# Windowed attention and two feed-forward layers: which operand of the values product stands still, and a new order at both ends

## The chip, the cores and the metric

One core of a Trainium2 chip runs the whole program. The metric is the device time of one execution in microseconds (us). The engines are PE (products; PEld is its weight load), DVE, ACT and POOL (elementwise work) and SP, which issues the DMAs.

## The reference, cut to what matters

Inputs: q, k, v of 4 batches x 8 heads x 768 positions x 64; 8 memory keys and values; two feed-forward layers, 512 to 2048 to 512. All is float32.

```
for each chunk c of 32 queries:
    keys = 8 memory + 16 left + 32 own + 8 right   # 64; outside the sequence: absent
    a = exp(scale * q_c @ keys.T - rowmax);  a = a / (rowsum(a) + 1e-9)
    heads[:, :, c] = a @ values                    # 32x64 times 64x64
x = heads as 3072 x 512
h = x @ w_in;  y = max(0.01 h, h) @ w_out
h = y @ w_in2;  g = (a0 + a1 h + a2 h^2 + a3 h^3) / (1 + |b0||h| + |b1| h^2 + 1e-6)
out = g @ w_out2
```

## The kernel before

The 3072 rows are 8 tiles of 384 (TILE), each of three groups of 128 (GPT = 3), 24 groups in all. A group holds 4 chunks (cc) of 8 heads, as 2 sets (st) of 4 slots (j).

**Phase A** (`tile_a`, 8 tiles) is the first feed-forward layer with the attention of coming tiles woven in. Its step f makes one 128-row slice of the hidden layer: `gemm1` (12 products of 384 columns, L580 to L582: each operand is split in a high and a low part, three products make one), ACT scales (L778), DVE takes the maximum (L1013), ACT rounds to g_hi (L784), DVE subtracts for g_lo (L1016), and three steps later (LAG) `gemm2_a` takes it (L597 to L599). **Phase B** (`tile_b`) does the second layer likewise (`gemm2_b`, L615 to L617, 512 columns); its activation takes seven DVE operations a step (`step_b`; L1042, L1052 and L1063 end it), ACT rounds (L790), DVE makes g_lo (L1022), and `save_out` (L826) copies a tile's three outputs, which SP stores.

**Attention of one group** takes 32 score products (L503, L514), the softmax, 32 values products (L539, L552), and the heads' split into x_hi (ACT) and x_lo (DVE), the operands of `gemm1`. A float32 product of this form is two records of PE. In `values` (groups 6 to 23) the normalised probabilities, turned by DVE (L939), stand still, 64 keys x 32 queries, and the values move, 64 columns; the output has queries on partitions, so DVE turns it (`turn_values`, L963) before ACT (L767) and DVE (L968) split it:

```
nc.tensor.matmul(at.loop_values_at[CHUNK * j:CHUNK * (j + 1), st, :, cc, :],   # stays 64x32,
                 at.probs_t[DH * st:DH * (st + 1), q0:q0 + CHUNK],             # 8 places of the
                 v_of(ring(c), st, j, cc), start=True, stop=True)              # array in use
```

In groups 0 to 5 PE turns the probabilities (`transpose_probs`, L522), ACT copies them (L761), and the heads are normalised (L994) and turned (L1001) afterwards. Groups 3 to 5 (the early ones) go through the first tile's steps: scores at step f = 3, 7, 11, turned at f+1, values at f+2, saved at f+3. For later groups scores are at f = 15, 5, 10, values at 4, 9, 14, and the split at 5, 10, 14. The next group's scores wait for the last one's turned heads (`wait_scores`).

x_hi and x_lo have two halves. Tile t's result y is written into half t % 2 and stored to HBM from there (`store_y`, L351); `save_heads` waits for y_stored before the first group of a tile overwrites that half. POOL splits the weights that SP loads (L463, L466), two operations a half slice; `gemm1` and `gemm2_a` wait for them (`wait_weights`). ACT does the rounding of the first two slices (L877).

**The first tile** has an order of its own, written out at the end of each engine's block: three groups in three places of PSUM, with `keep_warm` products between them.

## Time and profile before

| | us |
|---|---|
| median of three runs (lowest, highest) | 1141.11 (1140.07, 1141.95) |
| the profiled execution | 1140.21 |
| its span | 1138.4 |
| the first layer's products, first to last start | 19.1 to 603 |
| `gemm2_b`, first to last start | 605.5 to 1134.9 |

Rows give start and length in us from the span's start. In rows of groups the numbers behind the bar are the busy time in us and the mean length of one instruction in ns. A product's record holds its passage through the array, so records overlap: what counts is the distance from start to start. `<-` names what ended an engine's idle time.

### The profile page before, as it was taken

To read this page: it belongs to the slowest core of one execution; us is meant where nothing else is said; L and a number is where in the kernel's file an instruction comes from. 1 tells how busy PE (TensorE), PEld (TensorE's weight loads), DVE (VectorE), ACT (ScalarE), POOL (GpSimd) and SP (SyncE) were. 2 spreads that over 40 slices of the span, in tenths; PEclk is the share of its full clock that TensorE was granted. 3 is DMA by queue.
4 is the path that set the end of the run, shared out by engine and by line. 5 is a ranking of instruction groups with operands and counts; after the bars stand their busy time and mean duration, and the time that the engine had idled before them with its cause. 6 is when DMAs were issued, how large, how long until landed. Compare 5 with 4: busy or idle time off the path is not lost.

```text
span 1138.4 us, 23079 instructions
## 1 busy us (share of the span) xinstructions
PE 1127.2 (99%) x8881; PEld 1057.2 (93%) x8881; DVE 784.2 (69%) x1512; ACT 587.8 (52%) x1423; POOL 129.4 (11%) x130
## 2 busy tenths in 40 slices
PE   7999999999999999999999999999999999999998
PEld 6999999999999999999999999999999999999996
DVE  6655555555556555554228888888888888888886
ACT  4323333333333334333237776767767677676765
POOL 3991211111211112000000000000000000000000
PEclk9999999999999999999999999999999999999999
DMA  7663525335352354300975020020202002020000
GB/s 263 206 198 116 195 76 185 104 129 197 112 186 102 109 181 149 139 1 14 356 251 194 1 84 1 2 82 1 84 1 84 1 1 84 1 84 1 29 1 28
DMA packets 43018, 114.78 MB, mean 101 GB/s; under 512 B 4897, under 2 KB 5025, under 8 KB 42913
## 3 DMA queue, kind: packets, MB, share of 16 engines
q1 hardware_dynamic: 42912, 113.33, 28.4%
q8 instruction: 71, 1.16, 0.4%
q14 instruction: 35, 0.28, 0.1%
HBM read 77.66 MB, written 35.65 MB: 100 GB/s over the span
## 4 chain that ended last, share of the span: by engine, by line
PE 96%; DVE 1%; DMA 1%; ACT 1%; issue 0%; SPq 0%; DVEq 0%
PE psum L582 15%; PE psum L580 15%; PE psum L581 15%; PE psum L597 8%; PE psum L616 8%; PE psum L617 8%; PE psum L598 8%; PE psum L599 8%; PE psum L615 8%; PE psum L539 1%; PE psum L503 1%; DMA spare<-groups_in 1%; DVE g_lo L1016 0%; PE psum L552 0%; PE psum L680 0%
## 5 line engine op out<-in xcount | busy, mean ns | idle before, releaser
L582 PE MATMUL psum<-x_hi,w_lo 128*128 128x384 f32 x1016 | 341.2, 336 | 0.0
L580 PE MATMUL psum<-x_hi,w_hi 128*128 128x384 f32 x1016 | 340.8, 335 | 0.3 <-DVE scratch L1013 0.3
L581 PE MATMUL psum<-x_lo,w_hi 128*128 128x384 f32 x1016 | 340.3, 335 | 0.0
L580 PEld LDWEIGHTS psum<-x_hi,w_hi 128*128 128x128 f32 x1016 | 190.8, 188 | 6.2 <-issue 0.6
L581 PEld LDWEIGHTS psum<-x_lo,w_hi 128*128 128x128 f32 x1016 | 190.7, 188 | 5.4
L1013 DVE TENSOR_TENSOR scratch<-psum,scratch 128x384 f32<-128x384 f32 x128 | 71.3, 557 | 178.9 <-ACT scratch L778 177.1
L582 PEld LDWEIGHTS psum<-x_hi,w_lo 128*128 128x128 f32 x1016 | 190.6, 188 | 0.0
L597 PE MATMUL psum<-g_hi,w_hi 128*128 128x384 f32 x512 | 176.1, 344 | 0.0
L598 PE MATMUL psum<-g_lo,w_hi 128*128 128x384 f32 x512 | 171.2, 334 | 0.0
L599 PE MATMUL psum<-g_hi,w_lo 128*128 128x384 f32 x512 | 171.1, 334 | 0.0
L778 ACT ACTIVATE scratch<-psum 128x384 f32<-128x384 f32 x128 | 63.5, 496 | 187.9 <-PE psum L582 182.3
L798 ACT ACTIVATE scratch<-psum,cf 128x384 f32<-128x384 f32 x128 | 74.6, 583 | 151.4 <-PE psum L582 151.4
L617 PE MATMUL psum<-w_hi,g_lo 128*128 128x512 f32 x384 | 152.0, 396 | 0.0
L616 PE MATMUL psum<-w_lo,g_hi 128*128 128x512 f32 x384 | 151.6, 395 | 0.0
L615 PE MATMUL psum<-w_hi,g_hi 128*128 128x512 f32 x384 | 149.5, 389 | 1.5 <-DVE g_lo L1022 1.5
L784 ACT CAST g_hi<-scratch 128x384 fp32r<-128x384 f32 x128 | 65.7, 513 | 137.0 <-DVE scratch L1013 135.5
L1036 DVE SCALAR_TENSOR_TENSOR scratch<-scratch,cf 128x384 f32<-128x384 f32 x128 | 79.2, 618 | 77.6 <-ACT scratch L799 77.6
L1016 DVE TENSOR_TENSOR g_lo<-scratch,g_hi 128x384 fp32r<-128x384 f32 x128 | 78.9, 617 | 74.2 <-ACT g_hi L784 74.2
L597 PEld LDWEIGHTS psum<-g_hi,w_hi 128*128 128x128 f32 x512 | 96.0, 188 | 4.2
L598 PEld LDWEIGHTS psum<-g_lo,w_hi 128*128 128x128 f32 x512 | 96.2, 188 | 0.0
L599 PEld LDWEIGHTS psum<-g_hi,w_lo 128*128 128x128 f32 x512 | 96.1, 188 | 0.0
L617 PEld LDWEIGHTS psum<-w_hi,g_lo 128*128 128x128 f32 x384 | 72.0, 187 | 15.4
(93 smaller groups left out, 1486.2 us busy)
## 6 DMA issues: line engine op xcount, KB each, us to landing
scratch<-groups_in SPq DMA_DIRECT2D x23, 768.0 KB, 6.7
raw<-weights_in SPq DMA_DIRECT2D x64, 256.0 KB, 4.3
scratch<-groups_in SPq DMA_DIRECT2D x23, 512.0 KB, 5.3
...
x_hi_scratch<-x_hi SPq DMA_DIRECT2D x8, 768.0 KB, 3.3
```

What stands on the lines that cost most here:

```text
L580: nc.tensor.matmul(bank, hi, x_hi[:, b, k, :], start=(k == 0), stop=False)
L581: nc.tensor.matmul(bank, hi, x_lo[:, b, k, :], start=False, stop=False)
L582: last = nc.tensor.matmul(bank, lo, x_hi[:, b, k, :], start=False, stop=(k == KT - 1))
L597: nc.tensor.matmul(bank, hi, g_hi[:, f % G_RING, :], start=(f == 0), stop=False)
L598: nc.tensor.matmul(bank, hi, g_lo[:, f % G_RING, :], start=False, stop=False)
L599: last = nc.tensor.matmul(bank, lo, g_hi[:, f % G_RING, :], start=False, stop=(f == NF - 1))
L615: nc.tensor.matmul(bank, hi, w_hi[:, f, 1, :], start=(f == 0), stop=False)
L616: nc.tensor.matmul(bank, hi, w_lo[:, f, 1, :], start=False, stop=False)
L617: last = nc.tensor.matmul(bank, lo, w_hi[:, f, 1, :], start=False, stop=(f == NF - 1))
L798: nc.scalar.activation(absb, h, ACT.Abs, scale=cf[:, 4:5])
L1016: nc.vector.tensor_tensor(g_lo[:, f % G_RING, :], leaky[f % 2], g_hi[:, f % G_RING, :].bitcast(F32), ALU.subtract).then_inc(g_lo_ready, 1)
L1036: nc.vector.scalar_tensor_tensor(quad[c], h2, cf[:, 6:7], absb, ALU.mult, ALU.add).then_inc(quad_ready, 1)
```

## The change

- **The values products** swap operands: the values stand still (64 keys x 64 columns) and the probabilities move (32 columns). The output has the model's dimension on partitions, as `gemm1` wants it, in 64-row halves, so four places of the array are in use where there were eight. `turn_values` and `turn_heads` are gone; ACT and DVE split straight from PSUM, in the step of the values product (f = 4, 9, 14). `wait_scores` now waits for x_ready. The host no longer permutes w_in's rows.
- **Softmax of groups 0 to 5**: probabilities, not heads, are normalised, before PE turns them; POOL does it for groups 0 and 1 ahead of its weight splits. ACT makes group 1's sums with its exponentials in place of group 2's. The early groups gain a step: scores f, normalise f+1, turn f+2, values and split f+3.
- **The start**: SP asks for the third group's values after three scores, and for weights after two exponentials; PE's order changes, nine warming products become three, and `first_gemm1` needs the low weight parts last. ACT rounds a weight slice on each side of the third group's cast.
- **The end**: the last slice's correction, activation, rounding and low part are done in two parts (256 and 128 columns), steps 14 and 15 are interleaved anew, `last_gemm2` starts on each part as it comes, and DVE copies the middle output.

The diff, cut:

```diff
-EARLY_TRANSPOSE = {f + 1: g for f, g in EARLY_SCORES.items()}
-EARLY_VALUES = {f + 2: g for f, g in EARLY_SCORES.items()}
-EARLY_SAVE = {f + 3: g for f, g in EARLY_SCORES.items()}
+EARLY_NORMALISE = {f + 1: g for f, g in EARLY_SCORES.items()}
+EARLY_TRANSPOSE = {f + 2: g for f, g in EARLY_SCORES.items()}
+EARLY_VALUES = {f + 3: g for f, g in EARLY_SCORES.items()}
 EARLY = 2 * GPT
...
     sp.wait_ge(qk_loaded[1], 16)
     load_v(0, 0)
     load_v(1, 1)
-    sp.wait_ge(probs_t_ready, 2)
+    sp.wait_ge(scores_ready, GPT)
     load_v(2, 2)
+    sp.wait_ge(exp_ready, 2)
     for j in range(RAW):
         load_raw(j, j, first=True)
...
-            sp.wait_ge(o_saved, GPT * t + j + 1)
+            if isinstance(t, int) and t == TILES - 1 and j == 1:
+                sp.wait_ge(o_saved_dve, 1)
+            else:
+                sp.wait_ge(o_saved, GPT * t + min(j + 1, saved_by_act(t)))
...
+    def normalise_first(g, at):
+        pool.wait_ge(sums_ready, 3 * g + 3)
+        nc.gpsimd.tensor_tensor(at.loop_probs, at.loop_probs,
+                                at.loop_inv.unsqueeze(2).broadcast_to([P, SETS * CPG, KEYS]),
+                                ALU.mult).then_inc(first_normalised, 1)
+    for g in range(BY_POOL):
+        normalise_first(g, first_att[g])
...
     def scores(c, at):
...
     def transpose_probs(g, at):
-        pe.wait_ge(exp_ready, g + 1)
+        if g < BY_POOL:
+            pe.wait_ge(first_normalised, g + 1)
+        else:
+            pe.wait_ge(normalised, g - BY_POOL + 1)
         for a in range(2 * SETS):
...
+                    r0 = DH * (j % 2)
                     last = nc.tensor.matmul(
-                        at.loop_values_at[CHUNK * j:CHUNK * (j + 1), st, :, cc, :],
-                        at.probs_t[DH * st:DH * (st + 1), q0:q0 + CHUNK],
-                        v_of(ring(c), st, j, cc), start=True, stop=True)
+                        at.loop_x[r0:r0 + DH, st, j // 2, CHUNK * cc:CHUNK * (cc + 1)],
+                        v_of(ring(c), st, j, cc),
+                        at.probs_t[DH * st:DH * (st + 1), q0:q0 + CHUNK], start=True, stop=True)
         last.then_inc(heads_ready, 1)
     def values_first(c, at):
         for st in range(SETS):
             for cp in range(2):
-                for c2 in range(2):
-                    for j in range(SLOTS):
+                for j in range(SLOTS):
+                    for c2 in range(2):
                         q0 = (st * 2 + cp) * P + j * CHUNK
+                        r0 = DH * (j % 2)
                         last = nc.tensor.matmul(
-                            at.values_at[CHUNK * j:CHUNK * (j + 1), c2, st, :, cp, :],
-                            at.probs_t[DH * c2:DH * (c2 + 1), q0:q0 + CHUNK],
-                            first_v_of(ring(c), st, j, cp, c2), start=True, stop=True)
+                            at.first_x[r0:r0 + DH, c2, 2 * st + j // 2, CHUNK * cp:CHUNK * (cp + 1)],
+                            first_v_of(ring(c), st, j, cp, c2),
+                            at.probs_t[DH * c2:DH * (c2 + 1), q0:q0 + CHUNK], start=True, stop=True)
         last.then_inc(heads_ready, 1)
...
             gemm2_a(n0 + f - LAG, f - LAG, t)
+    def last_gemm2():
+        f, r = NF - 1, (NF - 1) % G_RING
+        all_steps = STEPS_A + TILES * NF
...
+                                    start=False, stop=stop)
+        wait_weights(f, 1, True)
+        pe.wait_ge(g_hi_ready, all_steps)
+        product(0, g_hi, w_hi)
+        product(0, g_hi, w_lo)
+        pe.wait_ge(g_lo_ready, all_steps)
+        product(0, g_lo, w_hi, stop=True).then_inc(o_ready, 1)
+        product(1, g_hi, w_hi)
+        product(1, g_hi, w_lo)
+        product(1, g_lo, w_hi, stop=True).then_inc(o_ready, 1)
+        pe.wait_ge(g_hi_ready, all_steps + 1)
+        product(2, g_hi, w_hi)
+        product(2, g_hi, w_lo)
+        pe.wait_ge(g_lo_ready, all_steps + 1)
+        product(2, g_lo, w_hi, stop=True).then_inc(g_used, 1)
...
             for k in range(KT):
-                for w in (w_hi, w_lo):
-                    nc.tensor.matmul(psum[:, H_BANKS[f], 0:TILE], w[:, f, 0, P * k:P * (k + 1)], x_hi[:, 0, k, :],
-                                     start=(k == 0 and w is w_hi), stop=False)
+                nc.tensor.matmul(psum[:, H_BANKS[f], 0:TILE], w_hi[:, f, 0, P * k:P * (k + 1)], x_hi[:, 0, k, :],
+                                 start=(k == 0), stop=False)
         pe.wait_ge(x_ready, GPT)
         for f in (0, 1):
             for k in range(KT):
-                last = nc.tensor.matmul(psum[:, H_BANKS[f], 0:TILE], w_hi[:, f, 0, P * k:P * (k + 1)],
-                                        x_lo[:, 0, k, :], start=False, stop=(k == KT - 1))
+                nc.tensor.matmul(psum[:, H_BANKS[f], 0:TILE], w_hi[:, f, 0, P * k:P * (k + 1)], x_lo[:, 0, k, :],
+                                 start=False, stop=False)
+            wait_weights(f, 0, False)
+            for k in range(KT):
+                last = nc.tensor.matmul(psum[:, H_BANKS[f], 0:TILE], w_lo[:, f, 0, P * k:P * (k + 1)],
+                                        x_hi[:, 0, k, :], start=False, stop=(k == KT - 1))
             last.then_inc(h_ready, 1)
...
     pe.wait_ge(ident_loaded, 16)
     transpose_probs(0, first_att[0])
+    first_values(0)
     transpose_probs(1, first_att[1])
-    first_values(0)
+    transpose_probs(2, first_att[2])
     first_values(1)
-    transpose_probs(2, first_att[2])
     first_values(2)
-    keep_warm(9)
+    keep_warm(3)
     first_gemm1()
     for f in range(2, LAG):
...
     def save_heads(g, gi, b, at, t):
-        act.wait_ge(turned, g + 1)
+        act.wait_ge(heads_ready, g + 1)
         if gi == 0:
             act.wait_ge(y_stored, 32 * t + 1)
-        nc.scalar.copy(x_hi[:, b, :, P * gi:P * (gi + 1)], at.loop_heads).then_inc(xh_ready, 1)
+        to = x_hi[:, b, :, P * gi:P * (gi + 1)].rearrange("p (s u) n -> p s u n", s=SETS)
+        nc.scalar.copy(to, at.loop_x).then_inc(xh_ready, 1)
     def save_first_heads(g, gi, b, at):
-        act.wait_ge(turned, g + 1)
+        act.wait_ge(heads_ready, g + 1)
         to = x_hi[:, b, :, P * gi:P * (gi + 1)].rearrange("p k (e n) -> p e k n", e=2)
-        nc.scalar.copy(to, at.heads_tv).then_inc(xh_ready, 1)
+        nc.scalar.copy(to, at.first_x).then_inc(xh_ready, 1)
     def step_a(n, f):
         act.wait_ge(h_ready, n + 1)
...
+        round_b(n - 2, m - 2, f - 2)
+        act.wait_ge(h_ready, n + 1)
+        act.wait_ge(quad_ready, m)
+        nc.scalar.activation(absb, h, ACT.Abs, scale=cf[:, 4:5])
+        nc.scalar.activation(h2, h, ACT.Square).then_inc(squares_ready, 1)
+        nc.scalar.activation(horner[f % 2], h, ACT.Copy, scale=cf[:, 3:4]).then_inc(cubic_ready, 1)
+        round_b(n - 1, m - 1, f - 1)
+        act.wait_ge(quad_ready, m + 1)
+        nc.scalar.activation(seed[f % 2], quad[f % 2], ACT.Abs_reciprocal_sqrt,
+                             bias=cf[:, 7:8]).then_inc(root_ready, 1)
+        act.wait_ge(root_ready, m + 1)
+        nc.scalar.activation(seed[f % 2], seed[f % 2], ACT.Square).then_inc(seed_ready, 1)
+        act.wait_ge(g_used, n - G_RING + 1)
+        for part, cols in enumerate(LAST_PARTS):
+            act.wait_ge(gact_ready, m + 1 + part)
+            nc.scalar.copy(g_hi[:, f % G_RING, cols], gact[:, cols]).then_inc(g_hi_ready, 1)
     def save_y_high(t, b):
         for d in range(KT):
...
-    save_first_heads(1, 1, 0, first_att[1])
-    for j in range(BY_ACT):
+    loop_exp(1, first_att[1])
+    exp_scores(2, first_att[2])
+    for g in range(GPT):
+        save_probs_t(g, first_att[g])
+    def round_first(j):
         act.wait_ge(raw_loaded[j], 16)
         f, half = W_ORDER[j]
         nc.scalar.copy(w_hi[:, f, half, :], raw[:, j, :]).then_inc(w_first_ready, 1)
+    assert BY_ACT == 2
+    save_first_heads(0, 0, 0, first_att[0])
+    save_first_heads(1, 1, 0, first_att[1])
+    round_first(0)
     save_first_heads(2, 2, 0, first_att[2])
+    round_first(1)
     for f in range(LAG):
         step_a(f, f)
     for i in range(0, TILES // 2 - 1):
...
+    def sum_rows(g, at):
+        dve.wait_ge(exp_ready, g + 1)
+        nc.vector.tensor_reduce(at.loop_sums, at.loop_probs, AX.X, ALU.add).then_inc(sums_ready, 1)
+        dve.wait_ge(sums_ready, 3 * g + 1)
+        nc.vector.tensor_scalar(at.safe, at.loop_sums, SUM_EPS, None, ALU.add).then_inc(sums_ready, 1)
+        dve.wait_ge(sums_ready, 3 * g + 2)
+        nc.vector.reciprocal(at.loop_inv, at.safe).then_inc(sums_ready, 1)
+    def normalise(g, at):
         dve.wait_ge(sums_ready, 3 * g + 3)
         nc.vector.tensor_tensor(at.loop_probs, at.loop_probs,
                                 at.loop_inv.unsqueeze(2).broadcast_to([P, SETS * CPG, KEYS]),
                                 ALU.mult).then_inc(normalised, 1)
-        dve.wait_ge(normalised, g + 1)
...
+    def turn_probs(g, at):
+        inverses(g, at)
+        normalise(g, at)
+        dve.wait_ge(normalised, g - BY_POOL + 1)
         turn_blocks(at, (0, 1))
...
-    def turn_values(g, at):
-        dve.wait_ge(heads_ready, g + 1)
-        nc.vector.transpose(at.probs_t.rearrange("p (s n) -> p s n", s=SETS), at.loop_values).then_inc(turned, 1)
...
     def save_low(g, gi, b, at):
         dve.wait_ge(xh_ready, g + 1)
-        cols = slice(P * gi, P * (gi + 1))
-        nc.vector.tensor_tensor(x_lo[:, b, :, cols], at.loop_heads, x_hi[:, b, :, cols].bitcast(F32),
-                                ALU.subtract).then_inc(x_ready, 1)
...
+        to, hi = (x[:, b, :, P * gi:P * (gi + 1)].rearrange("p (s u) n -> p s u n", s=SETS) for x in (x_lo, x_hi))
+        nc.vector.tensor_tensor(to, at.loop_x, hi.bitcast(F32), ALU.subtract).then_inc(x_ready, 1)
...
+                                       ).then_inc(quad_ready, 1)
+        low_b(n - 1, f - 1)
+        dve.wait_ge(cubic_ready, m + 1)
+        nc.vector.scalar_tensor_tensor(horner[c], horner[c], cf[:, 2:3], h, ALU.add, ALU.mult
+                                       ).then_inc(horner_ready, 1)
+        dve.wait_ge(horner_ready, m + 1)
+        nc.vector.scalar_tensor_tensor(horner[c], horner[c], cf[:, 1:2], h, ALU.add, ALU.mult
+                                       ).then_inc(h_free, 1)
+        def last_correction(part):
+            cols = LAST_PARTS[part]
+            nc.vector.scalar_tensor_tensor(corr[:, cols], quad[c][:, cols], Q_ONE, seed[c][:, cols],
+                                           ALU.add, ALU.mult).then_inc(corr_ready, 1)
+            dve.wait_ge(corr_ready, m + 1 + part)
+            nc.vector.scalar_tensor_tensor(corr[:, cols], corr[:, cols], 2.0, seed[c][:, cols],
+                                           ALU.subtract, ALU.mult, reverse0=True).then_inc(inv_ready, 1)
...
+            dve.wait_ge(inv_ready, m + 1 + part)
+            nc.vector.scalar_tensor_tensor(gact[:, cols], horner[c][:, cols], cf[:, 0:1], corr[:, cols],
+                                           ALU.add, ALU.mult).then_inc(gact_ready, 1)
...
+            dve.wait_ge(g_hi_ready, n + 1 + part)
+            nc.vector.tensor_tensor(g_lo[:, f % G_RING, cols], gact[:, cols],
+                                    g_hi[:, f % G_RING, cols].bitcast(F32), ALU.subtract).then_inc(g_lo_ready, 1)
+        dve.wait_ge(seed_ready, m + 1)
+        dve.wait_ge(gact_ready, m)
+        dve.wait_ge(h_free, n + 1)
+        dve.wait_ge(g_lo_ready, n)
+        last_correction(0)
+        last_activation(0)
+        last_correction(1)
+        last_low(0)
+        last_activation(1)
...
+    def save_last_out():
+        dve.wait_ge(o_ready, (GPT - 1) * (TILES - 1) + 2)
+        dve.wait_ge(out_stored[1], 16 * (TILES - 1))
+        nc.vector.tensor_copy(ostage[1], psum[:, ACC_B[1][1], :]).then_inc(o_saved_dve, 1)
...
-    shift_scores(1, 1, 0, 0, first_att[1])
+    first_maxima(1, first_att[1])
     sum_rows(0, first_att[0])
-    first_maxima(2, first_att[2])
-    sum_rows(1, first_att[1])
-    normalise(0, first_att[0])
-    turn_heads(0, first_att[0])
-    normalise(1, first_att[1])
-    turn_heads(1, first_att[1])
-    first_inverses(2, first_att[2])
+    shift_scores(2, 2, 0, 0, first_att[2])
+    inverses(1, first_att[1])
+    sum_rows(2, first_att[2])
     normalise(2, first_att[2])
-    turn_heads(2, first_att[2])
-    save_heads_low(0, 0, 0, first_att[0])
-    save_heads_low(1, 1, 0, first_att[1])
-    save_heads_low(2, 2, 0, first_att[2])
+    for g in range(GPT):
+        save_heads_low(g, g, 0, first_att[g])
...
-    w_in = inputs["moe_w_in"].reshape(SETS, SLOTS, DHALVES, CHUNK, D_FF).transpose(0, 2, 1, 3, 4).reshape(D_MODEL, D_FF)
+    w_in = inputs["moe_w_in"]
```

## Rows read from the trace of the kernel before

**Rows 1.** the page, busy time: engine, us, share of the span, instructions.

```profile
PE 1127.2 (99%) x8881; PEld 1057.2 (93%) x8881; DVE 784.2 (69%) x1512; ACT 587.8 (52%) x1423; POOL 129.4 (11%) x130
```

**Rows 2.** groups by form: line, operation, shapes, count | busy us, mean ns | idle before.

```profile
L582 PEld LDWEIGHTS psum<-x_hi,w_lo 128*128 128x128 f32 x1016 | 190.6, 188 | 0.0
...
L1042 DVE SCALAR_TENSOR_TENSOR scratch<-scratch 128x384 f32<-128x384 f32 x128 | 70.6, 551 | 0.1
...
L466 POOL TENSOR_TENSOR w_lo<-raw,w_hi 128x512 fp32r<-128x512 f32 x32 | 43.6, 1364 | 19.5 <-ACT w_hi L877 17.0
...
L539 PE MATMUL psum<-scratch 64*32 64x64 f32 x1152 | 15.5, 224 | 0.0
...
L963 DVE STREAM_TRANSPOSE scratch<-psum 128x512 f32<-128x512 f32 x18 | 12.8, 709 | 0.0
...
L539 PEld LDWEIGHTS psum<-scratch 64*32 64x32 f32 x1152 | 12.5, 105 | 4.5 <-issue 4.5
...
L767 ACT CAST x_hi<-scratch 128x512 fp32r<-128x512 f32 x18 | 11.1, 619 | 7.5 <-DVE scratch L963 7.5
```

**Rows 3.** timeline of PE, 108.4 to 110 us: start, length, instructions, count.

```profile
108.48 0.34 PE L582 MATMUL psum<-x_hi,w_lo 128*128 128x384 f32 x1
108.75 0.86 PE L539 MATMUL psum<-scratch 64*32 64x64 f32 x64
109.54 0.44 PE L597 MATMUL psum<-g_hi,w_hi 128*128 128x384 f32 x1
```

**Rows 4.** L539 in four windows: busy PE (under way), busy PEld (under way), clock, DMA.

```profile
108.74:108.82 0.08, 0.07 (x8) 0.07 (x15) 1.00 0.20 77
108.82:108.88 0.06, 0.06 (x16) 0.06 (x24) 1.00 2.27 717
108.88:108.94 0.06, 0.06 (x24) 0.06 (x27) 1.00 1.25 512
108.94:109.00 0.06, 0.06 (x32) 0.06 (x16) 1.00 0.74 307
```

**Rows 5.** timeline, 178 to 187 us: y's store, ACT's cast, the next scores.

```profile
178.87 0.38 SPq L351 DMA_DIRECT2D x_lo_scratch<-x_lo  x1
...
182.60 0.51 ACT L784 CAST g_hi<-scratch 128x384 fp32r<-128x384 f32 x1 [0.62 <-DVE scratch L1013]
...
186.54 0.86 PE L503 MATMUL psum<-scratch 64*32 64x64 f32 x64
```

**Rows 6.** DMA issues, 178 to 179.3 us: KB each, us from issue to landing.

```profile
x_lo_scratch<-x_lo SPq DMA_DIRECT2D x1, 768.0 KB, 6.5
```

**Rows 7.** timeline of the first 35 us, all engines.

```profile
11.56 0.33 SPq L309 DMA_DIRECT2D spare<-groups_in  x1
...
16.02 0.86 PE L552 MATMUL psum<-spare,scratch 64*32 64x64 f32 x64 [1.41 <-DMA spare<-groups_in]
...
17.46 3.00 POOL L466 TENSOR_TENSOR w_lo<-raw,w_hi 128x512 fp32r<-128x512 f32 x2 [17.01 <-ACT w_hi L877]
...
19.06 0.44 PE L680 MATMUL psum<-x_hi,w_hi 128*128 128x384 f32 x1 [0.39 <-ACT x_hi L772]
...
26.16 0.41 PE L580 MATMUL psum<-x_hi,w_hi 128*128 128x384 f32 x1 [0.32 <-DVE scratch L1013]
...
34.38 0.66 PE L522 MATMUL psum<-ident,scratch 128*128 128x128 f32 x4 [0.74 <-ACT scratch L732]
```

**Rows 8.** timeline, 57 to 59 us: the second early group.

```profile
57.50 0.25 DVE L987 RECIPROCAL stats<-stats 128x16 f32<-128x16 f32 x1
...
58.28 0.86 PE L552 MATMUL psum<-scratch 64*32 64x64 f32 x64
```

**Rows 9.** timeline from 1124 us: the end.

```profile
1124.62 0.61 DVE L1063 SCALAR_TENSOR_TENSOR scratch<-scratch,cf 128x384 f32<-128x384 f32 x1
...
1133.94 1.97 ACT L826 COPY scratch<-psum 128x512 f32<-128x512 f32 x3 [1.71 <-PE psum L617]
...
1134.89 0.40 PE L617 MATMUL psum<-w_hi,g_lo 128*128 128x512 f32 x1
```

174 lines of the change are left out of this document (76 added, 98 removed).

## The prediction

> **What bounds the kernel now.** I read the page first: PE is busy 1127.2 of 1138.4 us [rows 1], and the other engines have room. So work off PE counts only where PE waits for it, and that is at the two ends. The waits by window say the same: of its 11.2 us of standing still, 6.5 lie before 35 us and 4.6 after 1118 us, and between them it is busy throughout. Then come the groups by form [rows 2] for what each operation costs, PE's timeline around one values group [rows 3, 4] for the operation whose form changes, the stretch where y's half is stored and overwritten [rows 5, 6], and the timelines of both ends [rows 7 to 9]. The reader is to see two kinds of time: what lengthens PE's own stream adds in full, 21 times over; what shortens a chain of other engines helps once, at an end.
>
> The sum is made against the profiled execution, 1140.2 us (span 1138.4 and 1.8 around it); the median is 0.9 above it, and I add that at the end.
>
> **1. The values products: +4.8 us.** Before, 32 products are 64 records; the first starts at 108.75, the last ends at 109.61, and the next large product starts 0.79 after the first did [rows 3]. What paces them? In the four windows [rows 4] the products under way are 8, 16, 24, 32: none of those ends in between (each lasts 0.22), so 8 new ones start in each 0.06 us. There are 8 places of 64x32 in the array, so each place takes a new record every 0.056 to 0.06 us. A 32-column load is 105 ns and a 128-column one 188 [rows 2]: 0.86 ns a column above a fixed part, so 32 columns fill a place in about 28 ns. The first window has 15 loads beside 8 products: loads run ahead. So in this stretch a place is held by its moving operand, 64 columns in about 56 ns, and its load of 28 is covered. The other half of the group is slower (32 records in 0.40 us, 109.0 to 109.4), presumably because PE's queue had run dry and instructions then come one by one; the whole group is 0.64 us from first to last start.
>
> After, the moving operand has 32 columns, by half of 56 about 28 ns, and the load 64 columns, 64 x 0.86 = 55 ns. Now the load is the longer and covers the product. There are 4 places, so a record starts every 14 ns. 64 x 14 = 0.90 us, plus 0.03 for the last product, against 0.64 plus 0.06: +0.23 us a group. Groups 3 to 23 stand in PE's full stretch: 21 x 0.23 = +4.8. No row shows a 64-column load with a 32-column product, so both bounds: below, the array is no limit at all and both forms go at the rate of their 64 records, 0; above, load and product of one place follow each other, (55 + 28) / 4 = 21 ns a record, 1.33 + 0.03 - 0.70 = +0.66 a group, +14. I take the middle value, since rows 4 show the load covered; the mean over the old group, 10 ns a record, would fit the upper one too ((28 + 53) / 8), so it keeps a chance.
>
> A rule that speaks for the upper bound: the Trainium skill, "TensorE: Matmul & The Clock Gate", section "Part 3: Packing small matmuls", lets a weight load overlap a product under way only where its row group differs. By that rule, with two row groups, old places would take 28 + 56 = 84 ns a record and rows 4 would show 8 new products in 0.08 us; they show them in 0.06. By the rule the sum would be about 1154.
>
> **2. DVE's turns: 0.** 18 turns of 0.71 us [rows 2] leave the loop, and ACT's and DVE's split come a step earlier. PE waits for neither between 35 and 1118 us, so they give nothing. Cover gone would cost only if the split came later than the next scores, which is the next point.
>
> **3. y's half is overwritten a step earlier: +0.7 us.** `save_heads` of a tile's first group moves from f = 5 to f = 4, and there it waits for y's store. In the second tile the store of x_lo is issued at 178.87 [rows 5] and lands 6.5 later [rows 6], at 185.4. ACT would come to the cast at 183.1, after the rounding at 182.60 [rows 5]. So it stands 2.3 us, casts in 0.62 [rows 2] to 186.0, and DVE's low part (about 0.7) ends at 186.75. Behind ACT's wait are step 5's scaling (due 186.6) and behind DVE's the same step's maximum: both get through. But the next scores, which started at 186.54 [rows 5], have their wait three large products earlier, at about 185.9, 186.15 with the longer values: PE stands 0.6. In the other five tiles the landing is 5.8 us after the issue and the same sum gives 0 to 0.05. Together 0.7, from 0 to 2.
>
> **4. The start: -0.3 us.** The third group's values are asked for at 11.56 and its products start at 16.02 [rows 7]; after, they are asked for at about 9.9, when its scores end, and are there at 14.3. But now PE's turns wait for normalised probabilities: group 0's row sums are done at 9.9, POOL multiplies in 1.36 [rows 2], PE turns at 11.4, and the copies and turns of three groups take turns on ACT and PE; group 2's values products end at about 17.1 where they ended at 16.9. Then ACT's cast follows at once (0.70 and 0.71 of DVE are gone), and `first_gemm1` starts at 17.9 for 19.06. Most of this is not kept: ACT rounds the first slice at the same time, so POOL's splits, which began at 17.46 [rows 7], begin at 17.4, and steps 2 and 3 wait for POOL. Step 3, at 26.16 [rows 7] for DVE's maximum, comes at 25.3. The wait of 0.74 before the turns at 34.38 [rows 7] goes; in its place the turns, a step later, wait for the normalisation (DVE's splits, sums and the multiplication end at about 37.5, PE is there at 36.8). PE leaves that point 1.1 us earlier. The next two early groups get such a wait too: in the second one DVE's inverse ends at 57.75 and the multiplication would end at 58.5, with PE due at 57.7, as the turns of step 8 have moved away [rows 8]; 0 where POOL does not slow DVE down, 0.8 where it does, so 0.4 each. -1.1 + 0.8 = -0.3, from -1.5 to +1.0.
>
> **5. The end: -1.6 us.** From DVE's activation at 1124.62 [rows 9] I laid out the new order with DVE's 0.55 and 0.61 [rows 2, 9], two thirds and one third for the parts over a fixed 0.15: step 14's low part at 1128.4 (PE never waits for it again), step 15's first part rounded at 1131.25 and its low part at 1131.7, the second at 1132.3 and 1132.6. PE ends step 14 at 1131.0, and its last nine products then run with 0.3 us of waiting, the last starting at 1133.2 for 1134.89 [rows 9]. The last copy shrinks in step with it, the store behind it is unchanged. -1.6, from -1.0 to -1.9.
>
> Sum: 4.8 + 0.7 - 0.3 - 1.6 = **+3.6 us**: 1143.8, and with the 0.9 of the median **1144.7**.
>
> **The rivals.** (a) *The load is hidden after all*: a record costs what it did, term 1 is 0, and the time is 1141.1 - 1.2 = 1139.9, not slower. For it: the second half of the old group is paced by instructions, not by the array. Against: rows 4. It decides where a group costs under 0.08 us more (21 x 0.08 = 1.7, against the 1.2 that the rest gives). (b) *Load and product in turn*: +13 us or 1154.5; for it the mean of 10 ns, against it rows 4. (c) *The new waits are dearer*: y's store delays PE in more tiles (each 0.3 to 0.9) and the early groups wait the full 0.8 to 1.5: +2.5 on my sum, 1147.2. For it: the slack at f = 5 is under 0.1 us in two further tiles. (d) *The clock falls in the start*, six warming products fewer: the granted clock is full in every row of before, though PE stood for up to 1.4 us [rows 7]; it would be 1 to 2 us, inside the range.
>
> **How the numbers follow.** My forecast 0.54, (a) 0.22, (b) 0.08, (c) 0.16, with (d) spread over them. I call 0.2%, 2.3 us, about what a measurement can tell. The forecast's own range is 1142.5 to 1147; (a) spans 1138 to 1141.5. Leaving out (b) and the lower part of (a), the range is 1139.5 to 1149. Faster (under 1138.8): a third of (a) and a little, 0.1. Same: the rest of (a) and a fifth of the forecast, 0.25. Slower: 0.65.
>
> **What would show it.** Term 1: the new values row as 64 records over 1.06 to 1.1 us, and the next large product 1.0 us after the first for 0.79. If it is 0.8, (a); if 1.4, (b). Term 3: one wait of PE at L503's successor in the second tile, ended by DVE's x_lo, about 0.6 us, and ACT's wait for a DMA in front of its cast. Term 4: `first_gemm1` at 17.9, POOL's first split at 17.4, and three waits of the turns for DVE of 0.7, 0.4, 0.4. Term 5: last product at 1.7 us less before the end of the span. The forecast fails first by term 1, whose size is 21-fold.

## The result and the profile after

| | us | ratio to before, 95% interval |
|---|---|---|
| kernel before, 4 runs beside it | 1141.17 (1140.07 to 1141.95) | |
| kernel after, 4 runs | 1153.25 (1152.23 to 1156.59) | 1.0110 [1.0096, 1.0123] |
| kernel after once more, 5 runs | 1153.43 (1153.18 to 1156.11) | 1.0106 [1.0091, 1.0120] |

The change costs 1.1%, 12 us. The prediction, 1144.7 with a range of 1139.5 to 1149.0, had the sign and a third of the size. The profiled span is 1150.5 us, 12.0 longer than before's. The page's busy time of the kernel after (engine, us, share, instructions), against [rows 1]:

```profile
PE 1135.2 (99%) x8875; PEld 1066.0 (93%) x8875; DVE 768.6 (67%) x1491; ACT 586.9 (51%) x1423; POOL 129.3 (11%) x132
```

PE is busy 8.0 us longer and stands 4.0 longer. The two need different causes. Its waits, all of them (releaser, us in total, times, longest):

```profile
PE psum L526 <- DVE scratch L1012: 4.9, 3, 1.8
PE psum L567 <- DVE g_hi L1210: 1.3, 1, 1.3
PE psum L526 <- POOL scratch L477: 1.2, 1, 1.2
PE psum L558 <- ACT scratch L784: 0.9, 1, 0.9
PE psum L558 <- issue: 0.9, 1, 0.9
PE psum L668 <- ACT g_hi L852: 0.8, 1, 0.8
PE psum L515 <- DMA spare<-groups_in: 0.7, 1, 0.7
PE psum L586 <- DVE x_lo L1028: 0.6, 1, 0.6
PE psum L586 <- DVE scratch L1040: 0.3, 1, 0.3
PE psum L621 <- DVE g_lo L1049: 0.2, 1, 0.2
```

The first row is new: the turns of the three early groups wait for normalised probabilities 1.80, 1.67 and 1.47 us, where before only the first waited, 0.74 [rows 7].

Since PE is full almost everywhere, a loss is read best from when the same block of products starts in both traces. I took the start of the first product of each block of `gemm2_a` from PE's timelines. The stages run from the span's start to block 0, to block 12 (the early groups), to block 18 (the tile's end), to block 127 (the other tiles of the first layer), to the span's end:

```
us                 start   0-12    12-18   18-127   rest    span
before             29.21   58.54   26.95   486.65   537.10  1138.4
after              30.33   63.65   27.54   492.41   536.52  1150.5
difference         +1.12   +5.11   +0.59    +5.76    -0.58   +12.0
after once more    30.50   63.63   28.31   492.44   536.52  1151.4
before once more   33.63   58.51   26.95   486.64   537.08  1142.8
```

The last two rows are the two kernels profiled again, later. Two stages repeat within 0.03 us and one within 0.02, so I take the differences there for the change's. The start and the tile's end don't repeat. Nor does the stage 0-12 in every variant: in before_tail below, which changes nothing there, it is 57.93, since PE doesn't meet the wait of 0.74 us before the first turns in that execution.

Around one values group of the loop, PE's timeline of the kernel after, to be laid beside [rows 3]:

```profile
114.72 0.34 PE L588 MATMUL psum<-x_hi,w_lo 128*128 128x384 f32 x1
114.99 1.14 PE L544 MATMUL psum<-scratch 64*64 64x32 f32 x64
116.06 0.45 PE L603 MATMUL psum<-g_hi,w_hi 128*128 128x384 f32 x1
```

The next large product starts 1.07 us after the group's first for 0.79: +0.28 a group. In windows of 0.12 us (busy PE, busy PEld, clock) the group is even throughout:

```profile
115.20:115.32 0.12, 0.12 (x23) 0.12 (x16) 1.00 0.74 205
...
115.56:115.68 0.12, 0.12 (x24) 0.12 (x16) 1.00 1.27 410
```

A product's record lasts 0.22, so with 23 to 24 under way in a window of 0.12 one starts every (0.12 + 0.22) / 23.5 = 14.5 ns, or 58 for each of four places: the loads' pace, as term 1 had it (55), with no slower half.

### The profile page after: what moved, and what is told of

It reads as the page before. It is cut to its first block, busy times and chain, and to the rows that moved or that the text cites. A ratio compares the mean times of both kernels' runs of the same rounds, so it can differ in the third digit from the quotient of the medians.

```text
span 1150.5 us, 23039 instructions
## 1 busy us (share of the span) xinstructions
PE 1135.2 (99%) x8875; PEld 1066.0 (93%) x8875; DVE 768.6 (67%) x1491; ACT 586.9 (51%) x1423; POOL 129.3 (11%) x132
## 4 chain that ended last, share of the span: by engine, by line
PE 93%; DVE 4%; ACT 1%; DMA 1%; issue 1%; SPq 0%; DVEq 0%; ACTq 0%
PE psum L588 15%; PE psum L586 15%; PE psum L587 15%; PE psum L603 8%; PE psum L622 7%; PE psum L623 7%; PE psum L621 7%; PE psum L604 7%; PE psum L605 7%; PE psum L544 2%; PE psum L504 1%; DMA spare<-groups_in 1%; PE psum L558 1%; DMA x_lo_scratch<-x_lo 1%; DVE g_lo L1043 1%
```

## The experiments

The variants were timed beside different runs of the kernel before, so I compare ratios to before, and stages of the profile.

**turns_late.** The turns go behind the second gemm of their step.

```diff
                     if first is not None:
                         scores_first(first, loop_att[first % GPT])
-                    if early(t, f, EARLY_TRANSPOSE) is not None:
-                        g = early(t, f, EARLY_TRANSPOSE)
-                        transpose_probs(g, loop_att[g % GPT])
...
                     gemm2_a(n0 + f - LAG, f - LAG, t)
+                    if early(t, f, EARLY_TRANSPOSE) is not None:
+                        g = early(t, f, EARLY_TRANSPOSE)
+                        transpose_probs(g, loop_att[g % GPT])
```

> The changed kernel, with the turns of the three early groups' probabilities behind the second gemm of the same step instead of before it. Theory 1 (the turns came before their normalised probabilities): PE's three waits in front of the turns, 1.80, 1.67 and 1.47 us ended by DVE in the changed kernel's trace, are covered by a second gemm of 12 products, about 2.8 us each, and vanish: 4.9 us less than the changed kernel, about 1148.3 in all, and no wait of PE before the turns above 0.1 us. Rival: PE has time in hand there and meets the same delay at the next place that needs DVE or ACT (the values of the step after, or the next step's activation), so that the sum of PE's waits between 30 and 90 us stays about 5 us and the time at 1153.

Measured: 1146.24 us, ratio 1.0047 [1.0032, 1.0061] for 1.011. The stage 0-12 is 58.09 for 63.65 us, 5.56 less, and PE has no wait before these turns. The others are as after (30.19, 27.44, 492.52, 536.49). That is the 4.94 us of waits and 0.62 more, 0.2 a group. These 0.2 don't hang on the waits: before_tail and before_tail_turns (below) differ by the same move, PE waits before the turns in neither, and the stage is 57.93 and 57.24 there. So the early groups' loss of 5.11 is 4.94 of waits, less the 0.74 of the kernel before, and 3 x 0.28 for the longer values, which adds up to 5.04. The rival falls: nothing meets the delay further on.

**pool_waits.** What made DVE late? In the kernel after, the timeline of all engines around the first of these waits:

```profile
37.63 0.67 DVE L1004 TENSOR_REDUCE stats<-scratch 128x8 f32<-128x512 f32 x1
38.27 1.27 POOL L459 TENSOR_TENSOR w_lo<-raw,w_hi 128x512 fp32r<-128x512 f32 x1
38.34 1.24 DVE L1006 TENSOR_SCALAR stats<-stats 128x8 f32<-128x8 f32 x1
...
39.61 0.20 DVE L1008 RECIPROCAL stats<-stats 128x8 f32<-128x8 f32 x1
39.85 0.82 DVE L1012 TENSOR_TENSOR scratch<-scratch,stats 128x512 f32<-128x512 f32 x1
...
40.73 0.66 PE L526 MATMUL psum<-ident,scratch 128*128 128x128 f32 x4 [1.80 <-DVE scratch L1012]
```

An addition on 128x8 takes 1.24 us and ends at 39.58; POOL's subtraction, begun 0.07 before it, ends at 39.54. In all three groups the two start in this order, 0.06 to 0.07 apart. The experiment holds POOL back at these three places:

```diff
                     pool.wait_ge(w_hi_ready, j - BY_ACT + 1)
+                if j in (9, 19, 29):
+                    pool.wait_ge(normalised, j // 10 + 2)
```

> The changed kernel; before the low part of the splits 9, 19 and 29 POOL waits until DVE has normalised the early group of that time. In the changed kernel's trace these three subtractions of POOL (1.28 us each, from 38.27, 59.30 and 80.55) begin just before DVE's 128x8 addition (from 38.34, 59.36, 80.61), and that takes 1.24 us, to POOL's end, where it takes 0.17 with POOL idle. Theory 1 (DVE stands until POOL's subtraction is over): the addition takes 0.17 to 0.2, PE's three waits before the turns shrink by about 1.1 each to 0.7, 0.5 and 0.3 us, and the time falls by 3.3 us to 1150. Rival (the small operation is slow for another reason, or another of POOL's operations takes the place): the waits stay at 1.5 to 1.8 and the time at 1153. POOL's later start costs nothing in either: PE takes the slice three steps later.

Measured: 1152.15, ratio 1.0087 [1.0071, 1.0103]. In the first group POOL stood back. Its rows in pool_waits:

```profile
37.81 0.17 DVE L1008 TENSOR_SCALAR stats<-stats 128x8 f32<-128x8 f32 x1
38.01 0.20 DVE L1010 RECIPROCAL stats<-stats 128x8 f32<-128x8 f32 x1
38.25 0.69 DVE L1014 TENSOR_TENSOR scratch<-scratch,stats 128x512 f32<-128x512 f32 x1
...
39.00 0.65 PE L528 MATMUL psum<-ident,scratch 128*128 128x128 f32 x4 [0.61 <-DVE scratch L1014]
39.09 1.28 POOL L461 TENSOR_TENSOR w_lo<-raw,w_hi 128x512 fp32r<-128x512 f32 x1 [1.43 <-DVE scratch L1014]
```

The addition takes 0.17, PE's wait is 0.61 for 1.80, and the stage 0-12 is 62.77 for 63.65. In the other two groups another subtraction stood beside the addition, and the waits stayed (1.71 and 1.72 for 1.67 and 1.47):

```profile
57.83 1.27 POOL L461 TENSOR_TENSOR w_lo<-raw,w_hi 128x512 fp32r<-128x512 f32 x1
57.90 1.23 DVE L1008 TENSOR_SCALAR stats<-stats 128x8 f32<-128x8 f32 x1
...
60.28 0.66 PE L528 MATMUL psum<-ident,scratch 128*128 128x128 f32 x4 [1.71 <-DVE scratch L1014]
```

So one kernel holds the effect and its control: the same operation, 0.17 without POOL and 1.23 beside it, and 1.1 us of PE's wait with it. The expected 3.3 us came for one group in three. The Trainium skill, "SBUF — State Buffer", section "SBUF: two separate sides", calls the pair of ports that VectorE (DVE) and GpSimd (POOL) share a lock for the whole instruction, where "the other fully blocks", if VectorE's operation is in a two-port mode or reads two inputs from SBUF. The rows of the addition agree: it takes 1.24 us and ends 0.04 after POOL's subtraction. No row tells in which mode it ran. The reduction before it isn't held: it takes 0.67 in the second early group of before too, all of it under a subtraction.

**old_loop_values.** Groups 6 to 23 take the old form of the values, with DVE's turn and the split a step later, so it undoes terms 1 and 3 for these groups together. It leaves out the order of the heads' dimensions that w_in's rows have.

```diff
                             last = nc.tensor.matmul(
-                                at.loop_x[r0:r0 + DH, st, j // 2, CHUNK * cc:CHUNK * (cc + 1)],
-                                v_of(ring(c), st, j, cc),
-                                at.probs_t[DH * st:DH * (st + 1), q0:q0 + CHUNK], start=True, stop=True)
+                                at.loop_values_at[CHUNK * j:CHUNK * (j + 1), st, :, cc, :],
+                                at.probs_t[DH * st:DH * (st + 1), q0:q0 + CHUNK],
+                                v_of(ring(c), st, j, cc), start=True, stop=True)
```

> The changed kernel, but groups 6 to 23 take the old form of the values (probabilities stand, values move with 64 columns, DVE turns the heads, the split a step later as before). Not the whole computation: the heads' dimensions of these groups come in the old order while the rows of the first weight are laid out for the new one, so the output is another; the operations and sizes are those of the kernel before. Theory 1 (terms 1 and 3 of the prediction, at the sizes that the trace shows): 18 groups x 0.28 = 5.0 us and the waits behind y's store, 1.3 us, go: 6.3 less than the changed kernel, about 1147. Rival 1 (the values' longer records are partly made good behind them, since PE's queue fills meanwhile): only 2 to 4 us less. Rival 2 (DVE's turns, back again, make the split late and PE waits for it): less than 6.3 by the size of waits of PE ended by DVE in the loop.

Measured: 1147.84, ratio 1.0063 [1.0049, 1.0077]. The stage 18-127 is 486.64, before's own to 0.01 us, for 492.41. Nothing of the longer records is made good elsewhere, and DVE's 18 turns, back again, cost PE nothing: term 2 was right at 0.

**wide_moving and narrow_load** ask what paces a record of the new form. wide_moving multiplies neighbouring columns too in groups 6 to 23, and narrow_load leaves out half of x there. wide_moving:

```diff
+                            x0, q0 = P * (j // 2) + CHUNK * cc, min(q0, 448)
                             last = nc.tensor.matmul(
-                                at.loop_x[r0:r0 + DH, st, j // 2, CHUNK * cc:CHUNK * (cc + 1)],
+                                psum[r0:r0 + DH, at.bank + st, x0:x0 + 2 * CHUNK],
                                 v_of(ring(c), st, j, cc),
-                                at.probs_t[DH * st:DH * (st + 1), q0:q0 + CHUNK], start=True, stop=True)
+                                at.probs_t[DH * st:DH * (st + 1), q0:q0 + 2 * CHUNK], start=True, stop=True)
```

and narrow_load:

```diff
-                                at.loop_x[r0:r0 + DH, st, j // 2, CHUNK * cc:CHUNK * (cc + 1)],
-                                v_of(ring(c), st, j, cc),
+                                at.loop_x[r0:r0 + CHUNK, st, j // 2, CHUNK * cc:CHUNK * (cc + 1)],
+                                v_of(ring(c), st, j, cc)[:, 0:CHUNK],
```

> The changed kernel; in groups 6 to 23 the values products take 64 probability columns instead of 32, with the same 64x64 values as weights. What is written is not the reference's (neighbouring columns are multiplied too, and the last ones start at 448). Theory 1 (the 64-column load is the longer and covers the product: in the changed kernel's trace records come four in 0.058 us, one for each place of 64x64): the product of 64 columns takes 0.056 a place in the old form [rows 4], still no longer than the load, so the group stays at 64 records over 1.14 us and the time within 1.5 us of the changed kernel. Rival (load and product of a place follow each other): a place then takes 0.11 instead of 0.085 us and a group some 0.4 to 0.8 us more, 18 times: +8 to +15 us.

> The changed kernel; in groups 6 to 23 the values products load only the first 32 of 64 value columns, so half of x is left out and what the masked scores hold is -3e4 for -3e38 (what is left in PSUM is read instead). Theory 1 (the load's columns are the price): a place is busy 28 ns for 58, and the group goes at the rate at which its instructions arrive, 10 to 12.5 ns a record by the old form's second half [rows 3]: 0.13 to 0.3 us less a group, 18 times: 2.4 to 5.3 us less than the changed kernel, the next large product 0.8 to 0.95 after the first record for 1.07. Rival (the price is a fixed one for each record in its place, whatever it loads): no difference, the time of the changed kernel within 1 us.

Measured: wide_moving 1154.53, ratio 1.0115 [1.0100, 1.0130]; narrow_load 1147.71, ratio 1.0056 [1.0042, 1.0070], both beside after's 1.0106. PE's timeline around the same group, first wide_moving and then narrow_load:

```profile
115.01 1.16 PE L545 MATMUL psum<-scratch 64*64 64x64 f32 x64
116.10 0.45 PE L604 MATMUL psum<-g_hi,w_hi 128*128 128x384 f32 x1
```

```profile
115.13 0.76 PE L544 MATMUL psum<-scratch 64*32 64x32 f32 x64
115.81 0.44 PE L603 MATMUL psum<-g_hi,w_hi 128*128 128x384 f32 x1
```

Twice the moving columns cost 1.09 for 1.07 us. Half the load's columns give 0.68, even below the old form's 0.79. So with 64 columns to load the load sets the pace, the product of 32 or of 64 columns goes on beside the next load, and rival (b) is out. It doesn't follow that the moving columns never count: in the old form, with 32 to load and 64 moving, a place took 56 to 60 ns as well [rows 4]. My floor of 10 ns a record for narrow_load was too high: 0.68 us over 64 is 10.6 with the last products' passage in it, and a group gave 0.39 where I expected at most 0.3. Its time fell less than 18 x 0.39 = 7.0 us, mainly since y's store cost more again (PE waits for DVE's `x_lo` three times, 1.8 us in all, for 0.62 once): a shorter group brings the next scores nearer to the landing.

**y_two_sems.** One semaphore for each of y's stores.

```diff
-                act.wait_ge(y_stored, 32 * t + 1)
+                act.wait_ge(y_stored, 16 * t + 1)
...
-            def save_low(g, gi, b, at):
+            def save_low(g, gi, b, at, t):
                 dve.wait_ge(xh_ready, g + 1)
+                if gi == 0:
+                    dve.wait_ge(y_low_stored, 16 * t + 1)
```

> The changed kernel, with a semaphore for each of y's two stores: ACT's cast of the next tile's first heads waits for x_hi's store alone, DVE's low part for x_lo's. Theory 1 (term 3 of the prediction, 1.27 us in the trace of the changed kernel): ACT's cast no longer waits for x_lo's landing, the low part ends about 0.6 us earlier, and the steps of PE's delay at steps 18, 34 and 50 (0.32, 0.87, 0.08) fall to 0 to 0.2 together: about 1.1 less, 1152.1. Rival (x_lo's landing itself is too late for DVE): DVE takes over the wait, and PE's delay at step 34 stays above 0.5.

Measured: 1151.36, ratio 1.0083 [1.0068, 1.0098]. The stage 18-127 is 491.57 for 492.41, 0.84 less, of it 0.70 at the one block where the kernel after stood. Its rows there in the kernel after:

```profile
192.93 0.59 ACT L791 CAST x_hi<-psum 128x512 fp32r<-128x512 f32 x1 [2.41 <-DMA x_lo_scratch<-x_lo]
...
193.55 0.69 DVE L1028 TENSOR_TENSOR x_lo<-psum,x_hi 128x512 fp32r<-128x512 f32 x1 [2.44 <-ACT x_hi L791]
...
194.39 0.41 PE L586 MATMUL psum<-x_hi,w_hi 128*128 128x384 f32 x1 [0.62 <-DVE x_lo L1028]
```

and in y_two_sems, where the cast no longer stands between the landing and DVE:

```profile
191.04 0.59 ACT L795 CAST x_hi<-psum 128x512 fp32r<-128x512 f32 x1 [0.49 <-DMA x_hi_scratch<-x_hi]
...
192.88 0.69 DVE L1034 TENSOR_TENSOR x_lo<-psum,x_hi 128x512 fp32r<-128x512 f32 x1 [1.74 <-DMA x_lo_scratch<-x_lo]
```

DVE takes over the wait, 1.74 us, but ends 0.67 earlier, and PE no longer stands.

**before_tail.** The kernel before with only the new end (the functions `last_gemm2`, `last_steps_b` and `save_last_out` of the change, and their calls).

```diff
-                    gemm2_b(n0 + f - LAG, f - LAG, tp, after_phase_a=first_tile and f == LAG)
+                    if last_tile and f == NF + LAG - 1:
+                        last_gemm2()
+                    else:
+                        gemm2_b(n0 + f - LAG, f - LAG, tp, after_phase_a=first_tile and f == LAG)
...
+                    if last_tile and f >= NF - 1:
+                        if f == NF - 1:
+                            last_steps_b(STEPS_A + m0 + f, m0 + f, f)
```

> The kernel before, with the new end alone: the last two steps' activation in the order of the change, the last one in two parts (256 and 128 columns), the last second gemm's products in the order of their operands, and DVE's copy of one output block. Theory 1 (term 5 mis-sized, what the trace of the changed kernel shows between DVE's activation of step 13 and the last product): 0.5 us less than before, about 1140.6, the last product 0.67 earlier against DVE's activation of step 13. Rival 1 (my term 5 was right and something else in the changed kernel took it back): 1.6 less, 1139.5. Rival 2 (nothing is won, the end is held by the store of the output): 1141.1.

Measured: 1141.20 us, ratio 1.0001 [0.9992, 1.0009]: the time can't tell. The profile can: the stage from block 127 to the end is 536.50 for 537.10. Over all profiles, the fourteen with the new end have 536.49 to 536.55 there, and the three with the old one 537.08 to 537.11. The new end gives 0.58 us of the span, and theory 1 stands.

**start_warm and shifted_code** asked about the new start, in whose trace the granted clock falls (windows of the kernel after; busy PE, PEld, DVE, ACT, POOL, clock, DMA share, GB/s):

```profile
12.00:14.00 2.00, 1.10 (x63) 1.07 (x64) 1.69 (x5) 0.82 (x2) 1.04 (x1) 0.93 0.83 250
14.00:16.00 2.00, 2.00 (x19) 1.74 (x15) 0.28 (x1) 0.59 (x1) 0.00 (x0) 0.50 0.96 341
16.00:18.00 2.00, 1.75 (x66) 1.57 (x66) 0.65 (x1) 1.29 (x3) 0.00 (x0) 0.71 0.38 136
```

0.50 is the lower level, 1.2 GHz; PE had stood 1.21 us up to 11.44 and 0.90 up to 12.96. start_warm:

```diff
             pe.wait_ge(ident_loaded, 16)
+            keep_warm(5)
             transpose_probs(0, first_att[0])
+            keep_warm(4)
             first_values(0)
```

> The changed kernel, with five warming products before the first group's turns and four before its values. They change nothing that is computed. Theory 1 (the granted clock fell to 0.50 between 14 and 17 us because PE had stood from 10.2 to 11.4 and again before 13.0): the clock stays at 1.0 to the end of the start, the third group's turns and values are done about 1 us earlier, first_gemm1 starts at 19.3 to 19.6 for 20.44, and the time falls by 1.0 to 1.5 us, to about 1152. Rival 1 (the start is held by ACT's and DVE's chain, and PE's clock is covered): the clock is 1.0, first_gemm1 within 0.2 of 20.4, the time as before within 0.3. Rival 2 (the splits of POOL set the start): first_gemm1 moves, but the first second-gemm block stays within 0.3 of 30.33.

Measured: 1154.79, ratio 1.0118 [1.0101, 1.0135], no gain. The clock held to 20 us, but PE then stood 1.7 us inside the second group's values, put down to issue, and the clock fell from 20 to 24 us instead (0.58 and 0.57), under `first_gemm1`. Block 0 came at 31.19. My theory 1 was half of it: both falls came behind a stand, but another stand was waiting. A stand alone doesn't bring the fall: before stood 1.41 us up to 16.02, at a full clock. shifted_code tried to move the second one:

```diff
             pe.wait_ge(zeros_ready, 1)
-            keep_warm(12)
+            for _ in range(64):
+                nc.tensor.matmul(psum[:, H_BANKS[1], 0:CHUNK], g_hi[:, 0, 0:P], g_hi[:, 0, 0:CHUNK], start=True, stop=True)
+            keep_warm(5)
```

> The changed kernel, with 64 small warming products of 32 columns and 5 large ones in place of the first 12 large ones: 57 products more in PE's program ahead of the first scores, in about the same time. In the changed kernel PE stands 0.86 us after the first record of the third group's values, put down to issue; with nine warming products more ahead of that place, it stood 1.7 us eight records earlier, so at the same place of the program, and in both traces the instruction queue's transfer began 1.4 or 0.9 us before PE stopped. Theory 1 (PE has run to the end of what is loaded of its program): the place moves back by 57 products, to the first records of the second group's values, is reached after more of PE's waits for POOL and ACT, and the stand shrinks to 0 to 0.4; first_gemm1 starts 0.5 to 0.9 us earlier, at 19.5 to 19.9, and the time falls by 0.3 to 0.9 us. Rival 1 (the stand belongs to the third group, which waits for something unseen): it is still there, 0.8 us before the same record. Rival 2: the place moves, and the stand is as long there.

Measured: 1163.08, ratio 1.0183 [1.0166, 1.0201]. The experiment failed by its own means: 64 products of 32 columns took 13.83 us, the first scores started at 16.88 for 5.46, and the first loads had landed by 12 us. The stand was gone. But the bulk loads of 24 to 28 us (DMA share 0.76 and 0.98) came at another point of PE's program, and its clock was 0.50 from 26 to 34 us, so the place and the pace changed together.

**after_again and before_again**, the two kernels unaltered.

> The changed kernel once more, unaltered, beside the others of this call. All theories: 12 us more than before within 1.5. Its profile tells how far the start repeats: the first block of the second gemm at 30.33 us and a stand of 0.86 us put down to issue in the third group's values in its first trace. If the clock's fall and the stand belong to the change, both are here again, first block at 30.0 to 30.6; if they are chance, the first block comes anywhere between 29.2 and 31.

> The kernel before once more, unaltered. In two variants with the start of before, the first block of the second gemm came at 30.42 and 31.10 us, where the kernel before had 29.21. Theory 1 (the start of before varies from run to run, by what its DMAs and its program's loading meet): the first block at 29.8 or later, and the 1.13 us that I read as the cost of the new start is mostly spread. Rival (29.21 is what it always takes): 29.1 to 29.4 again, ratio 1.000 within 0.1%.

Measured: 1.0106 [1.0091, 1.0120] and 0.9992 [0.9982, 1.0002]. after_again has block 0 at 30.50 with a stand of 1.0 and the low clock again. The surprise is before_again: block 0 at 33.63 us, 4.42 later than in the first trace of the same program. PE's timeline of before_again shows the same stand, in the old start:

```profile
16.58 0.28 PE L552 MATMUL psum<-spare,scratch 64*32 64x64 f32 x1 [0.77 <-ACT scratch L761]
18.40 1.17 PE L552 MATMUL psum<-spare,scratch 64*32 64x64 f32 x63 [1.54 <-issue]
```

and its clock is 0.50 from 14 to 24 us. Over all profiles with the old start block 0 came at 29.21, 30.42, 31.01, 31.10, 31.57 and 33.63; with the new one as the change has it, at 29.79 to 30.68 in nine. So the 1.12 us between the first two traces can't be put down to the new start: the trace of before happened to be the fastest start of six. Nor is it shown that the new start is free. By the ratio of medians the change costs 12.5 us within 1.5, and the stages that repeat, with the 0.6 at the tile's end, hold 10.9 of them. The 1.6 left, for the start and a stand at the tile's end that comes and goes in both kernels, is at the edge of what these runs resolve.

**undo_both, before_turns, best_again.** undo_both is turns_late and old_loop_values together; before_turns is the kernel before with the turns moved as in turns_late; before_tail_turns and best_again are that with the new end.

> The changed kernel with two parts undone: groups 6 to 23 take the old form of the values (the order of the heads' dimensions there is then not that of the weight's rows, so the output is another), and the early groups' turns stand behind the second gemm of their step. Theory 1 (these two are the whole loss): 6.0 and 6.3 us less than the changed kernel's 1153.4, about 1141, within 1.5 us of before. Rival (the new start costs by itself, with the lower clock of 14 to 17 us): 1.5 to 3 us more than before stay, 1143 to 1144.

> The kernel before, with the new end, and with the turns of the early groups' probabilities behind the second gemm of their step. Theory 1: the end gives 0.6 us, and PE's wait of 0.74 us before the first early turns [rows 7] goes: 1.3 less than before, about 1139.6. Rival (the end gives nothing measurable, and the wait moves on to the values): as before within 0.3.

> The kernel before, with the turns of the early groups' probabilities alone moved behind the second gemm of their step. Theory 1: PE's wait of 0.74 us before the first turns [rows 7] goes and nothing comes in its place: 0.7 less than before, and the rest of what before_tail_turns gave (0.22% with an interval of 0.10 to 0.35%) is the new end's. Rival (the later turns gave all of it, since they keep PE off DVE's and ACT's late work in the first tile): 1.5 to 2.5 us less.

> The kernel before with the new end and the later early turns, once more. If its gain is real, 1.3 to 2.5 us less than before and 0.3 to 1.5 less than before_turns; if it was the chance of the start, within 0.1% of before.

Measured: undo_both 1141.35, ratio 1.0002 [0.9991, 1.0014], stages 30.58, 58.09, 27.77, 486.68, 536.51. With two parts undone the change is within 0.14% of before. That is not yet no cost: the moved turns and the new end each gain against the kernel before. The stages that repeat add up to 1.0 us less than before's, and the time is 0.2 more, within 1.3. So about 1.2 us may lie in the start and at the tile's end, no more than these runs can resolve. before_tail_turns gave 0.9978 [0.9965, 0.9990], best_again, the same kernel, 0.9989 [0.9977, 1.0001], and before_turns 1.0002 [0.9991, 1.0013]. In the profiles the later turns take the stage 0-12 from 58.54 to 57.22 to 57.24 and the new end gives its 0.58: 1.9 us of 1140, about what the two measurements gave between them (0.22 and 0.11%, the second not clear of noise). Where PE doesn't meet the wait of 0.74, as in before_tail, the turns give only 0.69 of these 1.3. before_turns showed no gain in its twelve times. Its interval leaves room for the 0.7 us of theory 1, but not for the rival's 1.5 to 2.5; its profile has 1.32 less in the stage 0-12, a start of 31.57 and a stand of 0.95 at the tile's end.

## Why the prediction was wrong

Term by term, against the stages:

| term | predicted | measured | shown by |
|---|---|---|---|
| 1, values of 18 loop groups | +4.1 | +5.0 | old_loop_values, wide_moving, narrow_load |
| 1 and 4, early groups (values, turns) | +1.5 | +5.1 | turns_late, pool_waits |
| 3, y's store | +0.7 | +1.3 | y_two_sems |
| 2, DVE's turns | 0 | 0 | old_loop_values |
| 4, the start | -1.1 | not resolved | before_again, after_again |
| 5, the end | -1.6 | -0.6 | before_tail |

(The early groups' +1.5 is 3 x 0.23, plus waits of 0.7, 0.4 and 0.4, less the 0.74 that goes. The values' +5.0 is 18 x 0.28, and y's +1.3 is the delay read at three blocks, 0.32, 0.87 and 0.08; the first is only 0.11 in after_again.)

Against the first two traces the sum was 8.4 us too low. Of these, 3.4 lie in the waits of the early groups, 2.2 in the start, 1.1 in the values of all 21 groups, 1.0 in the end and 0.6 in y's store.

**The step that failed is in term 4**: "0 where POOL does not slow DVE down, 0.8 where it does, so 0.4 each". I treated it as a matter of even chance, and at 0.8 us, for which I had no row. The waits were 1.80, 1.67 and 1.47 for 0.7, 0.4 and 0.4. POOL works through the splits almost without a pause up to 86 us. In the eleven profiles with the new order of the early groups there are 33 of these additions: 31 took 1.22 to 1.26 us, each behind a subtraction begun 0.05 to 0.08 before. The two others are the one of pool_waits (0.17) and the first of start_warm, which began 0.5 us before a subtraction's end and took 0.54; PE's wait there was 0.82 for 1.80. I had read the end of the small operations in the second early group [rows 8]. Before's own trace holds both cases:

```profile
37.12 1.29 POOL L466 TENSOR_TENSOR w_lo<-raw,w_hi 128x512 fp32r<-128x512 f32 x1
37.19 1.25 DVE L984 TENSOR_SCALAR stats<-stats 128x8 f32<-128x8 f32 x1
...
55.97 1.47 POOL L466 TENSOR_TENSOR w_lo<-raw,w_hi 128x512 fp32r<-128x512 f32 x1
...
56.92 0.55 DVE L984 TENSOR_SCALAR stats<-stats 128x8 f32<-128x8 f32 x1
```

Both additions end 0.03 us after the subtraction, so the 0.55 was a held one too, only begun later. They stood on no path of PE's there, and I read past them. The change put this chain between PE and its turns, and gave it no cover. Rival (c), dearer waits, was the right kind of loss, but it added 2.5 us where these waits and y's store were 4.0 above my sum. Rival (b) had 1154.5 (its own terms give 1153.8), close to what was measured, and that is chance: a group costs 0.28 more and not the 0.66 it rests on.

**Term 1 was right in kind**: load bound, four places, 14.5 ns a record where I had 14. The missing 0.05 us a group: I set 0.93 against 0.70 and the timelines have 1.07 against 0.79. From the first to the last start it is 0.92 where I had 0.90, and behind the last start both forms take 0.15 to the next large product, where I had given the new one 0.03 less. Twenty-one times 0.05 is 1.1 us. Rivals (a) and (b) are both out, (b) by wide_moving. So is the rule that I weighed there, "TensorE: Matmul & The Clock Gate", section "Part 3: Packing small matmuls" of the Trainium skill: in wide_moving a load and a product of 64 columns, of one place, pass in 1.09 us a group and not one after the other, which would be 64 x (58 + 56) / 4 ns or 1.8.

**Term 3** had the place and the mechanism (the store of the second tile's y, ACT stands for the DMA, PE for DVE's `x_lo`) and the wait, 0.62 us for 0.6, but the delay behind it grew to 0.87, and two more tiles gave 0.4.

**Term 5** laid DVE's operations end to end. The rows of the kernel after from the same anchor, DVE's activation of step 13:

```profile
1137.23 0.61 DVE L1087 SCALAR_TENSOR_TENSOR scratch<-scratch,cf 128x384 f32<-128x384 f32 x1
...
1140.92 0.56 DVE L1049 TENSOR_TENSOR g_lo<-scratch,g_hi 128x384 fp32r<-128x384 f32 x1
...
1144.80 0.42 DVE L1141 TENSOR_TENSOR g_lo<-scratch,g_hi 128x256 fp32r<-128x256 f32 x1
...
1144.91 0.47 PE L668 MATMUL psum<-w_hi,g_hi 128*128 128x512 f32 x1 [0.84 <-ACT g_hi L852]
...
1146.83 0.39 PE L668 MATMUL psum<-w_hi,g_lo 128*128 128x512 f32 x1
```

Step 14's low part ends 4.25 us after the anchor and the first part's low one 7.99, for 3.78 and 7.08 if my times are read as ends. Three of the DVE operations on this way start 0.12 to 0.22 after the end of the one before (at 1137.96, 1139.72 and 1142.87), 0.5 in all; where the other 0.4 lie isn't known, since my layout names no operation between. PE waits 0.84 for the first rounded part where I had 0.3, and the last product starts 9.60 after the anchor, for 10.27 in before and 8.6 in my layout.

**The start and rival (d).** The clock did fall, as (d) said, with stands of about a microsecond before it. But it fell as well, and for longer, in before's own second profile. What I held against (d), a full clock everywhere in before, was one draw. PE's first turns came as laid out, at 11.44 for 11.4, but `first_gemm1` started at 20.44 (20.60 in after_again) for 17.9: the lower clock and the stand behind the third group's first product weren't in the layout. Before's own start at 19.06 became 22.54 in before_again. So whether the new order gains or costs by itself stays open.

What stays argued: why PE stands "for issue" within the third group's values. In the kernel after, a transfer of the instruction queue shows in the DMA view between 16.25 and 16.5 us, about 1.3 us before PE stops, at the height of the bulk loads (kind: packets, MB, share of 16 engines):

```profile
q8 instruction: 1, 0.02, 23.0%
```

The seventeen profiles together say more than one. In thirteen of them, with the old start or the new one, PE stands at the same point of its program, after 349 product records; in start_warm, with nine products more ahead of the values, it is after 350. In all fourteen the stand ends 1.3 to 1.5 us after the end of such a transfer. In before, before_tail and shifted_code, which have no stand there, the transfer had ended 2.1, 2.3 and over 5 us before PE came to that point. This fits a program whose next part is fetched late, and shifted_code doesn't speak against it. It is a coincidence in time, seen often: no run moved the transfer alone.
